# Start and end of an attention plus two gated-layer kernel: new order of the first three chunks, last outputs stored bank by bank

## The chip, the cores and the metric

The kernel runs on one core of a Trainium2 chip. The time is the device time of one execution in microseconds (us); lower is better. A time is given as the median of several runs.

## The reference

```python
def _attn_ref(q, k, v, alpha):          # B, H, S, D = 4, 8, 768, 48
    for t in range(S):
        state = alpha[:, :, t, :, None] * state + np.einsum('bhd,bhe->bhde', k[:, :, t], v[:, :, t])
        y[:, :, t] = np.einsum('bhd,bhde->bhe', q[:, :, t], state)
# x = y as 3072 tokens x 384
x = (1 / (1 + np.exp(-(x @ w_gate)))) * (x @ w_val) @ w_out           # d_ff 1536
h = np.maximum(np.maximum(x @ w1, x @ w2), x @ w3)                     # d_ff 768
out = (h @ w_out2).astype(np.float32)
```

alpha lies between 0.8 and 1.0, so the kernel's general path (for an alpha further than 0.25 from 1) is compiled in but not executed for these inputs.

## The kernel before, in words

**Tiling.** The 3072 tokens are 24 chunks of 128 (CH) for the attention, 8 tiles of 384 (three chunks) for layer 1 and 6 tiles of 512 for layer 2. A chunk's attention is done in parallel form: running products of alpha (`scans`, `recips` on VectorE) scale q and k (`scale_qk`), TensorE computes `scores`, VectorE masks them (`masked`), TensorE transposes k (`transposes`), ScalarE copies the transposed keys to SBUF (`khs_copy`), TensorE forms the chunk's update of the state (`outer`) and the output y of the chunk (`attend`: the masked scores times v and, but for the first chunk of a batch, q times the state), VectorE updates the state (`new_state`), and ScalarE copies y to `x_raw` (`y_copy`). Part of y has the wrong rows; it is copied to `y_last` and moved by six small SBUF to SBUF transfers per tile (`move_last`, 24 KB each, two for each third k of the features, counted by `last_moved[k]`). Then every operand is split into a high and a low fp32r part (`x_split` on ScalarE gives `x_hi`, `x_rest` on VectorE gives `x_lo`), and every product is three passes of TensorE (`product`, L927, and `out1`, `out2`).

**Order.** Each engine has its own hand-written program; semaphores tie them. The attention of the chunks of tile T+1 lies between the products of tile T. Only the attention of the first three chunks (tile 0) has nothing beside it: it is the start of the kernel, L792 to L813 on VectorE, L1010 to L1022 on TensorE, L551 to L571 on ScalarE, L321 to L333 on SP (the queue that issues the loads). Layer 1 of tile 0 starts when `x_hi` of k = 0 is there.

**Places that the change touches.**

- `ps_y` (L108), the PSUM region of y, is one region for all chunks, across the two banks of `ps_pair`. So `attend` (L905) waits for `y_evac`: y of chunk 1 must be copied out before `attend(2, 0)` may write. `y_slot` (L901) picks a head's place in it.
- TensorE's order at the start (L1010 to L1022) is scores 0, transposes 0, outer 0, attend 0, scores 1, transposes 1, outer 1, scores 2, transposes 2, attend 1, outer 2, attend 2.
- ScalarE's order (L551 to L571) is key copy 0, `split_w1(0)`, y 0, `split_w1(1)`, key copy 1, `check(0)`, key copy 2, y 1, `check(1)`, y 2, two of the small moves (L565, from ScalarE's own queue, k = 1), `split_w1(2)`, and the three `x_split`. `check` (L538) tests alpha in two activations and gives `viol_done`.
- SP's order (L326 to L333) is w1 1 to 4, chunk 4, chunk 3, w1 5, the four moves of k = 0 and 2, w1 6 and on. `load_chunk(4)` waits for `y_done` 1 and `viol_done` 1, `load_chunk(3)` for `y_done` 2 and `viol_done` 2 (L236), `load_w1(5)` for `y_done` 2, and a chunk is two transfers, alpha (256 KB, L241) and the rest (704 KB, L242).
- VectorE's order (L806 to L811) is masked 1, new_state 1, masked 2, new_state 2, x_rest. Then `layer1` (L696) begins with `scans` and `recips` of chunk 3, ahead of the multiplication that gives the first h (L717).
- GpSimd makes the low parts of the weights (`split_first`, `split_w1`) and scales q and k of chunks 3 to 5 in between (L391 to L399).
- At the end, `out2` (L1029) does 12 matmuls: for each of the three passes n, all four banks s. `o_done` comes with the last one, then ScalarE copies the four banks (`o_copy`, L595) and SP stores each copy, 192 KB (L353 to L355).
- The general path, `general` and `slow_layers` on each engine, stands behind a branch on a flag.

Of the kernel before, what the change touches and what calls it, by code (L numbers as in the profile page):

```python
# [24 lines left out]
F32 = mybir.dt.float32  # L25
F32R = mybir.dt.float32r
I32 = mybir.dt.int32
ALU = mybir.AluOpType
# [35 lines left out]
def build(nc, att_in, vT, w1, w2, consts, y, out):  # L64
    with ExitStack() as ctx:
# [6 lines left out]
        def sem(name):  # L72
# [29 lines left out]
        ps_gate = pb("ps_gate", [P, 512])  # L102
        ps_val = pb("ps_val", [P, 512])
# [4 lines left out]
        ps_y = ps_pair[:, 512 - 2 * CH:512 + 2 * CH].rearrange("p (s t) -> p s t", s=PAIRS)  # L108
# [29 lines left out]
        o_evac, stored = sem("o_evac"), sem("stored")  # L138
        gen_qka, gen_v, gen_kv, gen_st, gen_prod = (sem(n) for n in ("gen_qka", "gen_v", "gen_kv", "gen_st", "gen_prod"))
        gen_sum, gen_row, gen_stored, gen_fix = sem("gen_sum"), sem("gen_row"), sem("gen_stored"), sem("gen_fix")  # L140
        s_w_in, s_w_hi, s_w_lo = sem("s_w_in"), sem("s_w_hi"), sem("s_w_lo")
        s_x_hi, s_x_lo, s_gate, s_val, s_sig, s_h = (
            sem(n) for n in ("s_x_hi", "s_x_lo", "s_gate", "s_val", "s_sig", "s_h"))
        s_h_hi, s_h_lo, s_out, s_mid = sem("s_h_hi"), sem("s_h_lo"), sem("s_out"), sem("s_mid")
        s2_w_in, s2_w_hi, s2_w_lo = sem("s2_w_in"), sem("s2_w_hi"), sem("s2_w_lo")
        s2_x_hi, s2_x_lo, s2_abc, s2_a, s2_ab, s2_h = (
            sem(n) for n in ("s2_x_hi", "s2_x_lo", "s2_abc", "s2_a", "s2_ab", "s2_h"))
        s2_h_hi, s2_h_lo, s2_out, s2_evac, s2_stored = (
            sem(n) for n in ("s2_h_hi", "s2_h_lo", "s2_out", "s2_evac", "s2_stored"))
# [42 lines left out]
        def arrived(eng, sems, Cs, i):  # L192

            if Cs == 2:
                eng.wait_ge(sems[2], 16)
            elif Cs < 2:
                eng.wait_ge(sems[Cs], 16)
            else:
                eng.wait_ge(sems[Cs % 2], (Cs // 2 + Cs % 2 + 3 * i) * 16)

# [31 lines left out]
        def _(sp):  # L232
# [58 lines left out]
            def slow_layers():  # L291
                for f in range(NF1):
                    if f > 0:
                        sp.wait_ge(s_w_hi, f)
                        sp.wait_ge(s_w_lo, f)
                    sp.dma_start(inbuf[:, 0:W1C], w1[f]).then_inc(s_w_in, 16)
                with sp.Fori(0, B) as b:
                    for half in (0, 1):
                        T = b * 2 + half
                        sp.wait_ge(s_x_lo, T * KT + 1)  # L300
                        for k in range(KT):
                            for r in (0, 1):
                                (p, n0), (pl, nl) = head_at(r, k), head_at(r, KT)
                                for n, (row, src) in enumerate((
                                        (ODD * r, y[b * PAIRS + p, n0, :, half * TOK:(half + 1) * TOK]),
                                        (ODD * r + D, y[b * PAIRS + pl, nl, GAP * k:GAP * (k + 1),
                                                        half * TOK:(half + 1) * TOK]))):
                                    sp.dma_start(x_raw[row:row + (GAP if n else D), k, :], src).then_inc(gen_fix, 16)
                sp.wait_ge(s_out, TILES * NF1 + 1)
                for j in range(NF2):  # L310
                    if j > 0:
                        sp.wait_ge(s2_w_hi, j)
                        sp.wait_ge(s2_w_lo, j)
                    sp.dma_start(inbuf[:, INC:INC + W2C], w2[j]).then_inc(s2_w_in, 16)
                sp.sem_inc(s2_stored, 16)
                with sp.Fori(0, TILES2) as T:
                    sp.wait_ge(s2_evac, T * SUB + 2 * SUB)
                    sp.dma_start(out[T], stage_out).then_inc(s2_stored, 16)
                sp.wait_ge(s2_stored, TILES2 * 16 + 16)
# [94 lines left out]
        def _(act):  # L414
# [13 lines left out]
            def y_copy(Cs, i):  # L428
# [6 lines left out]
                t = slice(c * CH, (c + 1) * CH)  # L435
# [59 lines left out]
            def slow_layers():  # L495
                act.sem_inc(s_sig, 1)
                act.sem_inc(s_mid, KT)
                for f in range(NF1):
                    act.wait_ge(s_w_in, 16 * (f + 1))
                    copy(w_hi[:, f * W1C:(f + 1) * W1C], inbuf[:, 0:W1C]).then_inc(s_w_hi, 1)  # L500
                with act.Fori(0, TILES) as T:
                    act.wait_ge(gen_fix, T * (4 * KT * 16) + 4 * KT * 16)
                    act.wait_ge(s_out, T * NF1 + 1)
                    for k in range(KT):
                        copy(x_hi[:, k, 0:TOK], x_raw[:, k, :]).then_inc(s_x_hi, 1)
                    for f in range(NF1):
                        act.wait_ge(s_gate, T * NF1 + f + 1)
                        act.wait_ge(s_h, T * NF1 + f + 1)
                        nc.scalar.activation(act_sb[:, :], ps_gate[:, 0:TOK], ACT.Sigmoid).then_inc(s_sig, 1)
                        act.wait_ge(s_h, T * NF1 + f + 2)  # L510
                        act.wait_ge(s_out, T * NF1 + f + 1)
                        copy(h_hi[:, 0, 0:TOK], h_sb[:, :]).then_inc(s_h_hi, 1)
# [3 lines left out]
                for j in range(NF2):  # L516
                    act.wait_ge(s2_w_in, 16 * (j + 1))
                    copy(w_hi[:, j * W2C:(j + 1) * W2C], inbuf[:, INC:INC + W2C]).then_inc(s2_w_hi, 1)
                act.sem_inc(s2_a, 1)
                act.sem_inc(s2_evac, SUB)  # L520
                with act.Fori(0, TILES2) as T:
                    act.wait_ge(s2_out, T * NF2 + 1)
                    act.wait_ge(s_mid, TILES * KT + KT)
                    for k in range(KT):
                        copy(x_hi[:, k, :], mid_tile2(T, k)).then_inc(s2_x_hi, 1)
                    for f in range(NF2):
# [3 lines left out]
                        act.wait_ge(s2_h, T * NF2 + f + 2)  # L530
                        act.wait_ge(s2_out, T * NF2 + f + 1)
                        copy(h_hi[:, 0, :], h2).then_inc(s2_h_hi, 1)
# [27 lines left out]
            check(1, 0)  # L560
# [32 lines left out]
            layer1(TILES - 1, 0, False, True, {LAST_READ[j] + 2: split_w2(j) for j in range(NF2)})  # L593

# [32 lines left out]
            o_copy(TILES2 - 1)  # L627
# [7 lines left out]
        def _(dve):  # L635
# [105 lines left out]
            def slow_layers():  # L741
                dve.sem_inc(s_h, 1)
                dve.sem_inc(s_x_lo, 1)
                dve.sem_inc(s2_h, 1)
                for f in range(NF1):
                    dve.wait_ge(s_w_hi, f + 1)
                    a = slice(f * W1C, (f + 1) * W1C)
                    nc.vector.tensor_tensor(w_lo[:, a], inbuf[:, 0:W1C], w_hi[:, a].bitcast(F32),
                                            ALU.subtract).then_inc(s_w_lo, 1)
                with dve.Fori(0, TILES) as T:  # L750
                    for k in range(KT):
                        dve.wait_ge(s_x_hi, T * KT + k + 1)
                        nc.vector.tensor_tensor(x_lo[:, k, 0:TOK], x_raw[:, k, :], x_hi[:, k, 0:TOK].bitcast(F32),
                                                ALU.subtract).then_inc(s_x_lo, 1)
                    for f in range(NF1):
                        dve.wait_ge(s_val, T * NF1 + f + 1)
                        dve.wait_ge(s_sig, T * NF1 + f + 2)
                        nc.vector.tensor_tensor(h_sb[:, :], act_sb[:, :], ps_val[:, 0:TOK], ALU.mult).then_inc(s_h, 1)
                        dve.wait_ge(s_h_hi, T * NF1 + f + 1)
                        nc.vector.tensor_tensor(h_lo[:, 0, 0:TOK], h_sb[:, :], h_hi[:, 0, 0:TOK].bitcast(F32),  # L760
                                                ALU.subtract).then_inc(s_h_lo, 1)
                for j in range(NF2):
                    dve.wait_ge(s2_w_hi, j + 1)
                    a = slice(j * W2C, (j + 1) * W2C)
                    nc.vector.tensor_tensor(w_lo[:, a], inbuf[:, INC:INC + W2C], w_hi[:, a].bitcast(F32),
                                            ALU.subtract).then_inc(s2_w_lo, 1)
                with dve.Fori(0, TILES2) as T:
                    for k in range(KT):
                        dve.wait_ge(s2_x_hi, T * KT + k + 1)
                        nc.vector.tensor_tensor(x_lo[:, k, :], mid_tile2(T, k), x_hi[:, k, :].bitcast(F32),  # L770
                                                ALU.subtract).then_inc(s2_x_lo, 1)
                    for f in range(NF2):
                        dve.wait_ge(s2_a, T * NF2 + f + 2)
# [410 lines left out]
```

## Time and profile before

| what | value |
|---|---|
| median of 3 runs | 874.21 us (873.68 to 874.39) |
| the profiled execution, its own time | 872.64 us |
| span of its profile | 870.8 us |
| TensorE (PE) busy | 847.7 us, 97% |
| VectorE, ScalarE, GpSimd busy | 353.5, 279.3, 114.1 us |
| instructions recorded | 14019 |

The span runs from the first to the last instruction of the profiled execution; 1.84 us of its own time lie around it. PE, DVE, ACT and POOL are TensorE, VectorE, ScalarE and GpSimd; PEld is TensorE's weight load, which runs beside its matmuls. SPq and ACTq are the issuing of transfers on the two queues. A name such as L922 is a line of the code above; L416 is the copy helper of ScalarE, used by many steps.

### The profile page before, as it was taken

Reading aid. Unit: us, or ns where it says so; the run is one execution under the profiler, and the core shown is the slowest. Engines: PE = TensorE matmul, PEld = TensorE weight load, DVE = VectorE, ACT = ScalarE, POOL = GpSimd, SP = SyncE. Lnnn points to the kernel's source line nnn. Section 1 sums busy time; section 2 is a strip of 40 time slices with the busy share of each in tenths; the row PEclk is TensorE's granted clock in tenths of the full one; section 3 lists DMA queues with packets and bytes.
Section 4 is the critical chain, followed back from the end, with each engine's and each line's share of the span. In section 5 each row is a group of like instructions: output and inputs, shape, how many; then the busy total and the mean of one; then the engine's idle time right before and its main releaser. Section 6 shows DMA issues by size and latency. Waiting matters only on the chain.

```text
span 870.8 us, 14019 instructions
## 1 busy us (share of the span) xinstructions
PE 847.7 (97%) x5565; PEld 786.1 (90%) x5565; DVE 353.5 (41%) x660; ACT 279.3 (32%) x520; POOL 114.1 (13%) x88
## 2 busy tenths in 40 slices
PE   5699999999999999999999999999999999999997
PEld 4599999999999999999999999988888888888886
DVE  7364354364274265255255322232323232232321
ACT  3364433333343333333333334421312122131211
POOL 1266121021012011012011004400000000000000
PEclk9999999999999999999999999999999999999999
DMA  7350210200111111021021022100100100000001
GB/s 279 124 209 1 99 46 1 99 18 30 54 44 47 40 59 47 8 91 47 5 93 47 1 80 78 69 1 1 37 1 0 36 0 36 0 36 0 36 0 39
DMA packets 14452, 42.17 MB, mean 48 GB/s; under 512 B 1984, under 2 KB 5952, under 8 KB 14400
## 3 DMA queue, kind: packets, MB, share of 16 engines
q1 hardware_dynamic: 14336, 41.38, 13.4%
q8 instruction: 39, 0.64, 0.3%
q14 instruction: 13, 0.11, 0.0%
q10 hardware_dynamic: 64, 0.05, 0.0%
HBM read 35.52 MB, written 4.72 MB: 46 GB/s over the span
## 4 chain that ended last, share of the span: by engine, by line
PE 97%; DVE 1%; DMA 1%; issue 0%; ACT 0%; SPq 0%; DVEq 0%; ACTq 0%
PE ps_out L959 18%; PE ps_gate L934 17%; PE ps_val L934 17%; PE ps_gate L940 9%; PE ps_val L940 9%; PE ps_out L1041 6%; PE ps_sc L934 6%; PE ps_pair L922 3%; PE ps_sc L940 3%; PE ps_sc L886 3%; PE ps_pair L1041 2%; PE ps_pair L918 1%; PE ps_pair L870 1%; PE ps_sc L896 1%; DMA x_raw<-x_raw 1%
## 5 line engine op out<-in xcount | busy, mean ns | idle before, releaser
L934 PE MATMUL ps_gate<-x_hi,w_hi 128*128 128x384 f32 (+1 forms) x396 | 139.7, 353 | 7.0 <-ACT x_hi L416 7.0
L934 PE MATMUL ps_val<-x_hi,w_hi 128*128 128x384 f32 (+1 forms) x396 | 140.6, 355 | 0.0
L934 PE MATMUL ps_gate<-x_hi,w_lo 128*128 128x384 f32 (+1 forms) x396 | 139.1, 351 | 0.0
L934 PE MATMUL ps_val<-x_hi,w_lo 128*128 128x384 f32 (+1 forms) x396 | 138.7, 350 | 0.0
L717 DVE TENSOR_TENSOR h_sb<-act_sb,ps_val 128x384 f32<-128x384 f32 x96 | 53.0, 552 | 169.1 <-PE ps_val L940 168.1
L940 PE MATMUL ps_gate<-x_lo,w_hi 128*128 128x384 f32 (+1 forms) x396 | 118.1, 352 | 0.0
L940 PE MATMUL ps_val<-x_lo,w_hi 128*128 128x384 f32 (+1 forms) x396 | 117.1, 349 | 0.0
L416 ACT ACTIVATE h_hi<-h_sb 128x384 fp32r<-128x384 f32 x96 | 50.4, 525 | 150.2 <-DVE h_sb L717 150.1
L462 ACT ACTIVATE act_sb<-ps_gate 128x384 f32<-128x384 f32 x96 | 47.2, 491 | 132.5 <-PE ps_gate L940 132.5
L934 PEld LDWEIGHTS ps_gate<-x_hi,w_hi 128*128 128x128 f32 x396 | 74.7, 189 | 10.6 <-issue 7.4
L836 DVE TENSOR_TENSOR probs<-probs,ps_val 128x512 f32<-128x512 f32 x36 | 24.7, 687 | 137.8 <-PE ps_val L940 137.8
L693 DVE TENSOR_TENSOR h_lo<-h_sb,h_hi 128x384 fp32r<-128x384 f32 x96 | 58.1, 605 | 52.0 <-ACT h_hi L416 52.0
L934 PEld LDWEIGHTS ps_val<-x_hi,w_hi 128*128 128x128 f32 x396 | 74.7, 189 | 4.4
L934 PEld LDWEIGHTS ps_val<-x_hi,w_lo 128*128 128x128 f32 x396 | 74.7, 189 | 4.4
L940 PEld LDWEIGHTS ps_gate<-x_lo,w_hi 128*128 128x128 f32 x396 | 73.4, 189 | 5.1
L934 PEld LDWEIGHTS ps_gate<-x_hi,w_lo 128*128 128x128 f32 x396 | 74.8, 189 | 3.2
L940 PEld LDWEIGHTS ps_val<-x_lo,w_hi 128*128 128x128 f32 x396 | 73.1, 188 | 4.2
L959 PE MATMUL ps_out<-h_hi,w_hi 128*128 128x384 f32 x288 | 67.9, 343 | 0.0
L959 PE MATMUL ps_out<-h_hi,w_lo 128*128 128x384 f32 x288 | 65.6, 335 | 0.0
L959 PE MATMUL ps_out<-h_lo,w_hi 128*128 128x384 f32 x288 | 65.4, 334 | 0.0
L369 POOL TENSOR_TENSOR inbuf<-inbuf,decay 112x512 f32<-112x512 f32 x21 | 27.1, 1292 | 288.5 <-DVE decay L645 284.8
L416 ACT ACTIVATE h_hi<-probs 128x512 fp32r<-128x512 f32 x36 | 22.8, 633 | 130.5 <-DVE probs L840 130.4
(113 smaller groups left out, 1242.2 us busy)
## 6 DMA issues: line engine op xcount, KB each, us to landing
inbuf<-att_in SPq DMA_DIRECT2D x23, 704.0 KB, 5.1
mid<-w SPq DMA_DIRECT2D x12, 576.0 KB, 7.3
inbuf<-att_in SPq DMA_DIRECT2D x23, 256.0 KB, 2.7
inbuf<-w SPq DMA_DIRECT2D x6, 768.0 KB, 4.3
out<-inbuf SPq DMA_DIRECT2D x5, 768.0 KB, 3.5
x_raw<-x_raw SPq DMA_DIRECT2D x46, 24.0 KB, 1.9
out<-inbuf SPq DMA_DIRECT2D x4, 192.0 KB, 2.4
mid<-att_in SPq DMA_DIRECT2D x1, 704.0 KB, 8.5
```

The lines of the kernel that those rows point to most:

```text
L369: nc.gpsimd.tensor_tensor(att(buf(Cs), Q), att(buf(Cs), Q), decay[0:PR, par], ALU.mult).then_inc(qh_done, 1)
L416: return nc.scalar.activation(o, i_, ACT.Copy)
L462: nc.scalar.activation(act_sb[:, :], ps_gate[:, 0:TOK], ACT.Sigmoid).then_inc(sig_done, 1)
L693: nc.vector.tensor_tensor(h_lo[:, f % 2, 0:w], h, h_hi[:, f % 2, 0:w].bitcast(F32), ALU.subtract).then_inc(lo_done, 1)
L717: nc.vector.tensor_tensor(h_sb[:, :], act_sb[:, :], ps_val[:, 0:TOK], ALU.mult).then_inc(h_done, 1)
L836: nc.vector.tensor_tensor(act2, act2, ps_val[:, :], ALU.max).then_inc(ab_done, 1)
L886: ins = mm(bank[:, p * CH:(p + 1) * CH], att(buf(Cs), K, r)[:, p, :], att(buf(Cs), Q, r)[:, p, :], start=True, stop=True)
L922: ins = mm(y_slot(p, n), v_cols(buf(Cs), (2 * p + n) * D, D), probs_of(Cs, i)[:, PAIRS * n + p, :], start=(first and p < 2), stop=True, sk ...
L934: mm(bank, w_at(half, f, c + k * P, total=total), x_hi[:, k, 0:w], start=(k == 0 and half == 0), stop=False)
L940: return mm(bank, w_at(0, f, c + k * P, total=total), x_lo[:, k, 0:w], start=False, stop=(k == KT - 1))
L959: ins = mm(ps_out[:, m, 0:TOK], w_at(wh, f, 2 * DM + m * P), h[:, f % 2, 0:TOK], start=(f == 0 and n == 0), stop=(f == NF1 - 1 and n == 2))
L1041: ins = mm(out_bank[s][:, 0:DM], h[:, f % 2, s * P:(s + 1) * P], w_at(wh, f, 3 * DM, DM, W2C), start=(f == 0 and n == 0), stop=(f == NF2 - ...
```

## The change

The edits:

1. y of chunk 1 gets its own banks (`ps_gate`, `ps_val`, now one tensor `ps_gv`), so `attend` of the first tile waits for no y copy but `attend(2)` for the one of chunk 0; the wait of `attend` for `khs_done` stays only outside the first tile, as before.
2. TensorE's `attend(0, 0)` goes behind scores and transposes of chunk 1. ScalarE's key copy 1 goes ahead of y 0. VectorE's `new_state(1)` goes behind the masks of chunk 2.
3. SP issues the four small moves ahead of chunk 3 and w1 5; ScalarE does `check(1)` behind its two moves (it was ahead of y 2), and `split_w1(2)` behind the three `x_split`.
4. The last `out2` runs bank by bank: three matmuls of a bank, then the next bank, each bank with its own count of `o_last`; ScalarE copies each bank on its count.
5. The general path's `slow_layers` are rewritten with loops and plain fp32 products (not executed here, and left out of the diff below); the kernel has 12 semaphores fewer for it and one more, `o_last`.

```diff
-        ps_gate = pb("ps_gate", [P, 512])
-        ps_val = pb("ps_val", [P, 512])
+        ps_gv = pb("ps_gv", [P, 2 * 512])
+        ps_gate, ps_val = ps_gv[:, 0:512], ps_gv[:, 512:1024]
...
-        ps_y = ps_pair[:, 512 - 2 * CH:512 + 2 * CH].rearrange("p (s t) -> p s t", s=PAIRS)
...
+        def y_banks(Cs, i):
+
+            two = ps_gv if isinstance(i, int) and Cs == 1 else ps_pair
+            return two[:, 512 - 2 * CH:512 + 2 * CH].rearrange("p (s t) -> p s t", s=PAIRS)
...
@@ SP @@
             load_chunk(4, 0)
+            move_last(0, (0, 2))
             load_chunk(3, 0)
-            load_w1(RING - 3)
-            move_last(0, (0, 2))
-            for f in range(RING - 2, NF1):
+            for f in range(RING - 3, NF1):
                 load_w1(f)
...
@@ ScalarE @@
             act.wait_ge(consts_in, 16)
+            khs_copy(1, 0)
             y_copy(0, 0)
             split_w1(1)
-            khs_copy(1, 0)
             check(0, 0)
             khs_copy(2, 0)
             y_copy(1, 0)
-            check(1, 0)
             y_copy(2, 0)
             act.wait_ge(y_evac, CPT - 1)
             act.wait_ge(last_evac, 1)
             for r in (0, ODD):
                 act.dma_start(x_raw[r + D:r + D + GAP, 1, :],
                               y_last[r + GAP:r + 2 * GAP, :]).then_inc(last_moved[1], 16)
-            split_w1(2)
+            check(1, 0)
             act.wait_ge(y_evac, CPT)
             for k in range(KT):
                 act.wait_ge(last_moved[k], 32)
                 x_split(0, k, x_raw[:, k, :])
+            split_w1(2)
...
+            def o_copy_last():
+                act.wait_ge(stored, 16 * (TILES2 - 1))
+                for s in range(SUB):
+                    act.wait_ge(o_last, s + 1)
+                    copy(stage_out[:, s, :], out_bank[s][:, 0:DM]).then_inc(o_evac, 1)
...
-            o_copy(TILES2 - 1)
+            o_copy_last()
...
@@ VectorE @@
             masked(1, 0, 0)
             masked(1, 0, 1)
-            new_state(1, 0)
             masked(2, 0, 0)
             masked(2, 0, 1)
+            new_state(1, 0)
             new_state(2, 0)
...
@@ TensorE @@
-                if not (isinstance(i, int) and Cs == 0):
+                if not (isinstance(i, int) and Cs < CPT):
                     pe.wait_ge(y_evac, C)
-                if not (isinstance(i, int) and Cs < CPT):
                     pe.wait_ge(khs_done, C + 1)
+                elif Cs == 2:
+                    pe.wait_ge(y_evac, 1)
...
             outer(0, 0)
-            attend(0, 0)
             scores(1, 0)
             transposes(1, 0)
+            attend(0, 0)
             outer(1, 0)
...
-            out2(TILES2 - 1, NF2 - 1)
+            pe.wait_ge(h2_hi_done, TILES2 * NF2)
+            pe.wait_ge(h2_lo_done, TILES2 * NF2)
+            f = NF2 - 1
+            for s in range(SUB):
+                for n, (h, wh) in enumerate(((h_hi, 0), (h_hi, 1), (h_lo, 0))):
+                    ins = mm(out_bank[s][:, 0:DM], h[:, f % 2, s * P:(s + 1) * P],
+                             w_at(wh, f, 3 * DM, DM, W2C), start=False, stop=(n == 2))
+                ins.then_inc(o_last, 1)
```

## Rows read from the trace of the kernel before

**Rows 1.** The page, part 2: busy tenths of TensorE in 40 slices of 21.8 us.
```profile
PE   5699999999999999999999999999999999999997
```

**Rows 2.** Chain of waits, 0 to 60 us, in order: start us, us, what.
```profile
13.56 1.95 PE ps_pair L922 x16
...
19.09 0.88 PE ps_sc L896 x10
19.97 2.01 PE ps_out L886 x16
21.98 0.94 PE ps_out L870 x4
22.92 1.03 PE ps_pair L918 x16
...
25.83 0.64 PE ps_out L896 x16
...
27.18 1.11 PE ps_pair L918 x16
...
30.22 0.27 ACT x_raw L416
...
30.84 0.64 SPq L263
...
36.46 0.53 ACT x_hi L416
37.12 1.62 PE ps_gate L934 x4
...
40.34 1.28 PE ps_val L934 x4
...
42.53 0.69 PE ps_gate L934 x4
...
57.25 1.01 PE ps_pair L922 x16
```

**Rows 3.** Timeline, 0 to 40 us: start us, us, engine, line, operation.
```profile
11.79 0.88 PE L896 MATMUL ps_out<-inbuf,khs 128*48 128x48 f32 x16 [0.63 <-ACT khs L416]
...
17.63 0.68 DVE L790 TENSOR_TENSOR mid<-mid,rdec 112x512 f32<-112x512 f32 x1
...
25.89 1.20 ACT L416 ACTIVATE x_raw<-ps_pair 48x512 f32<-48x512 f32 x2 [2.38 <-PE ps_pair L922]
27.11 0.72 ACT L542 ACTIVATE inbuf<-inbuf,cst 128x512 f32<-128x512 f32 x1
...
28.49 0.19 ACT L545 ACTIVATION_READ_ACCUMULATOR inbuf<-inbuf,cst 128x1 f32 x1
...
32.42 1.16 ACT L416 ACTIVATE w_hi<-mid 128x1152 fp32r<-128x1152 f32 x1 [0.64 <-issue]
```

**Rows 4.** Tile x_raw, 26 to 37 us: landing of its six moves.
```profile
DMA to landing us min/median/max: 3.8/4.6/5.0
```

**Rows 5.** Tile x_raw, 80 to 240 us: landing of 18 later moves.
```profile
DMA to landing us min/median/max: 1.8/1.9/3.5
```

**Rows 6.** Transfers issued 26 to 37 us: KB each, median us to landing.
```profile
inbuf<-att_in SPq DMA_DIRECT2D x1, 256.0 KB, 2.6
x_raw<-x_raw ACTq DMA_DIRECT2D x2, 24.0 KB, 4.8
```

**Rows 7.** Timeline of VectorE, 26 to 100 us.
```profile
38.42 1.36 DVE L645 TENSOR_TENSOR_SCAN decay<-inbuf,zero 112x128 f32<-112x128 f32 x4
...
42.57 0.55 DVE L717 TENSOR_TENSOR h_sb<-act_sb,ps_val 128x384 f32<-128x384 f32 x1 [1.09 <-PE ps_val L940]
```

**Rows 8.** Chain of waits, 862 to 871 us.
```profile
865.84 0.49 ACT inbuf L416
```

**Rows 9.** Stores to out and waits of SP, 860 to 871 us.
```profile
L355 SPq DMA_DIRECT2D out<-inbuf x4: 354/438/458, 866.4 to 867.7; - x4
...
SPq L65 <- DMA out<-inbuf: 2.2, 1, 2.2
```

More of the change, by code:

```diff
@@ L291, in slow_layers @@
             def slow_layers():
[L292 to L314, printed above, removed]
+                with sp.Fori(0, TILES) as T:
+                    b, t0 = T // 2, T % 2 * TOK
+                    sp.wait_ge(s_out, T * NF1 + 1)
+                    for k in range(KT):
+                        for r in (0, 1):
+                            (p, n), (pl, nl) = head_at(r, k), head_at(r, KT)
+                            sp.dma_start(x_raw[ODD * r:ODD * r + D, k, :],
+                                         y[b * PAIRS + p, n, :, bass.ds(t0, TOK)]).then_inc(gen_fix, 16)
+                            sp.dma_start(x_raw[ODD * r + D:ODD * r + D + GAP, k, :],
+                                         y[b * PAIRS + pl, nl, GAP * k:GAP * (k + 1), bass.ds(t0, TOK)]).then_inc(gen_fix, 16)
+                    with sp.Fori(0, NF1) as f:
+                        sp.wait_ge(s_out, T * NF1 + f + 1)
+                        sp.dma_start(w_slow, w1[f]).then_inc(s_w_in, 16)
@@ L315, in slow_layers @@
                 sp.sem_inc(s2_stored, 16)
                 with sp.Fori(0, TILES2) as T:
+                    with sp.Fori(0, NF2) as f:
+                        sp.wait_ge(s2_out, T * NF2 + f + 1)
+                        sp.dma_start(w2_slow, w2[f]).then_inc(s2_w_in, 16)
                     sp.wait_ge(s2_evac, T * SUB + 2 * SUB)
@@ L521, in slow_layers @@
                 with act.Fori(0, TILES2) as T:
[L522 to L526, printed above, removed]
+                    with act.Fori(0, NF2) as f:
                         act.wait_ge(s2_abc, T * NF2 + f + 1)
@@ L762, in slow_layers @@
[L762 to L766, printed above, removed]
-                with dve.Fori(0, TILES2) as T:
[L768 to L773, printed above, removed]
+                with dve.Fori(0, TILES) as T:
+                    with dve.Fori(0, NF1) as f:
+                        g = T * NF1 + f
+                        dve.wait_ge(s_val, g + 1)
+                        dve.wait_ge(s_sig, g + 2)
+                        dve.wait_ge(s_out, g + 1)
+                        nc.vector.tensor_tensor(h_sb[:, :], act_sb[:, :], ps_val[:, 0:TOK], ALU.mult).then_inc(s_h, 1)
@@ new lines, in slow_layers, with whole, step1, step2 @@
+            def slow_layers():
+                def whole(bank, w, c, x):
+                    for k in range(KT):
+                        ins = mm(bank, w[:, c + k * P:c + (k + 1) * P], x(k), start=(k == 0), stop=(k == KT - 1))
+                    return ins
+                def step1(T, f):
+                    g, first = T * NF1 + f, isinstance(f, int)
+                    pe.wait_ge(s_w_in, g * 16 + 16)
+                    pe.wait_ge(s_sig, g + 1)
+                    whole(ps_gate[:, 0:TOK], w_slow, 0, lambda k: x_raw[:, k, :]).then_inc(s_gate, 1)
+                    pe.wait_ge(s_h, g + 1)
+                    whole(ps_val[:, 0:TOK], w_slow, DM, lambda k: x_raw[:, k, :]).then_inc(s_val, 1)
+                    pe.wait_ge(s_h, g + 2)
+                    for m in range(KT):
+                        ins = mm(ps_out[:, m, 0:TOK], w_slow[:, 2 * DM + m * P:2 * DM + (m + 1) * P], h_sb[:, :],
+                                 start=first, stop=True, skip_group_check=True)
+                    ins.then_inc(s_out, 1)
+                def step2(T, f):
+                    G, first = T * NF2 + f, isinstance(f, int)
+                    pe.wait_ge(s2_w_in, G * 16 + 16)
+                    pe.wait_ge(s2_h, G + 1)
+                    whole(ps_gate[:, :], w2_slow, 0, lambda k: mid_tile2(T, k))
+                    whole(ps_val[:, :], w2_slow, DM, lambda k: mid_tile2(T, k))
+                    whole(ps_sc[:, :], w2_slow, 2 * DM, lambda k: mid_tile2(T, k)).then_inc(s2_abc, 1)
+                    pe.wait_ge(s2_h, G + 2)
+                    for s in range(SUB):
+                        ins = mm(out_bank[s][:, 0:DM], h2[:, s * P:(s + 1) * P], w2_slow[:, 3 * DM:4 * DM],
+                                 start=first, stop=True, skip_group_check=True)
+                    ins.then_inc(s2_out, 1)
@@ L1118, in _ @@
+                    step2(T, 0)
+                    with pe.Fori(1, NF2) as f:
+                        step2(T, f)
             pe.wait_ge(flag_ready, 1)
```

111 lines of the change are left out of this document (24 added, 87 removed).

## The prediction

> **What bounds the kernel now.** I read the page's slices first [rows 1]: TensorE is busy in nine tenths or more from the third slice to the last but one. Between about 44 and 863 us it is the bound, and no edit touches what it does there. Only the start (until layer 1 begins) and the last few us can change, so I read the chain of waits for both, in order of time.
>
> At the start the chain is on TensorE from the masks of chunk 0 to the end of `attend(2)` [rows 2]. Then come y copy, the issue of a small move, its landing (until 36.4), `x_split` at 36.46 and the first product at 37.12. So the start has two parts: TensorE's attention work with its holes, and the road of the last y rows by way of a transfer. At the end the chain is last matmul, four copies [rows 8], four stores, landing [rows 9].
>
> **Durations against medians.** The sum is made against the profiled execution, 872.64 us (span 870.8 and 1.84 around it). That is 1.57 below the median of the three runs; I subtract the same gain from 874.21.
>
> **Part 1, TensorE's order (edits 1 and 2).** `outer(0)` ends at 11.79 + 0.88 = 12.67 [rows 3]. Before, TensorE then waits for the masks until 13.56, later as long for key copy 1 as it did for key copy 0 (0.63 [rows 3]), and from 26.47 to 27.18 for the y copy of chunk 1, which `attend(2)` needed [rows 2]. In the new order its work after 12.70 is: scores 2.01, transposes 0.94, attend 1.95, outer 0.88, scores 2.01, transposes 0.94, attend with state 25.83 - 22.92 = 2.91, outer 0.64, attend 30.22 - 27.18 = 3.04 [rows 2]. (Scores and transposes of chunk 1 have the shapes of chunk 2.) Sum 15.32, end 28.02 where it was 30.22: **2.2 us earlier**, if no wait is left. I go through them:
> - scores 1 needs k of chunk 1, scaled before 12.67 (VectorE masks chunk 0 behind it and is done before 13.56).
> - Key copy 1 now runs beside `attend(0)` (from 15.7, done 16.3); outer 1 starts at 17.6.
> - scores 2 would start at 18.48; k of chunk 2 is scaled at 17.63 + 0.68 = 18.31 [rows 3]. Cover 0.17 us, the thinnest one; each us that VectorE is later costs a us.
> - Key copy 2: ScalarE has y 0 (1.20), w1 1 (1.16) and check 0 (1.57) between 17.6 and 21.6 [rows 3]; transposes 2 end at 21.4, the copy is done at 22.2, outer 2 needs it at 24.35.
> - `new_state(1)` moves behind the masks of chunk 2 (21.9, or 22.7 if GpSimd slows VectorE there) and ends by 23.5; attend(2) needs it at 24.98. Edit at nothing, cover 1.5 us.
> - chunk 4's load starts 1 us later, since `check(0)` ends at 21.6; its 960 KB are through by about 27, ahead of the moves.
>
> **Part 2, the moves (edit 3).** From the end of `attend(2)` to the first SP move it takes 30.84 - 30.22 = 0.62, so the moves issue from 28.64. ScalarE spends 32.42 - 30.84 = 1.58 until its two issues are over [rows 2, 3], so until 30.22, and then has `check(1)`: 28.49 + 0.19 - 27.11 = 1.57 [rows 3], until 31.8. For the landing: before, the six moves took 3.8 to 5.0 [rows 4], while chunk 3 and w1 5 (1.5 MB) were issued directly ahead. Later moves with nothing ahead land in 1.9, 1.8 to 3.5 [rows 5]. I take 1.9, since after the edit nothing is queued ahead either. k = 0 is there at 28.64 + 0.64 + 1.9 = 31.2; k = 2 at 30.6 + 1.9 = 32.5. So `x_split` 0 starts when `check(1)` ends, at 31.8 instead of 36.46: **4.66 us earlier in all** (2.2 of it part 1). The check in that place costs 0.6 against the landing at 31.2. With landings of 3.5, it starts at 32.8 (gain 3.7).
>
> Here a rule speaks against this reading. The trace shows ScalarE's own moves, on the other queue, landing in 4.8, as late as SP's [rows 6]. The Trainium skill, "DMA: Bandwidth & Descriptors", section "Queues, rings and completion order", says that a transfer engine takes turns between queues packet by packet; by that alone ScalarE's two moves should not have stood behind SP's bulk, so something else (their small rows) would have made them slow, and they would stay slow. By the rule the gain of this part is nil (first rival); by the later moves it is the one above.
>
> What is passed by the moves: SP issues chunk 3 only after `check(1)`, at 31.85, and w1 5 behind it. Alpha of chunk 3 lands after 2.6 [rows 6], at 34.5. VectorE ends `x_rest` at 38.42 - 4.66 = 33.8 and waits 0.7. It was idle 1.09 before the first h [rows 7], so h is not late. If it were: h was done at 43.12 [rows 7], and the value product of f = 1, which is the first to wait for it, comes nine matmuls of 0.17 after 42.53, at 44.1 [rows 2], so another 1.0 is free. Alpha may land until 33.8 + 1.09 + 1.0 = 35.9. Cost 0, bound 1 us. w1 5 is first read at f = 5, several steps later. `split_w1(2)` behind the x_splits ends by 34.5 and GpSimd's low part some 3 us later; f = 2 comes a whole step after f = 1, which starts at 42.53 - 4.66 = 37.9. Nothing.
>
> **Clock.** Layer 1 starts at half pace: four matmuls take 1.28 at 40.34 and 0.69 at 42.53 [rows 2], so the 4.5 us to 41.6 cost some 2.1 more than at full pace. The attention before it is at half pace too (1.95 against 1.01 at 57.25 [rows 2]). The profile's granted clock reads full all along, so it is the pitch that tells. I keep the 2.1; this stretch may be shorter or longer, from 0 to 4.2, and I allow 1 us either way.
>
> **Part 3, the end (edit 4).** Before, the copies start at 865.84 after the last matmul, SP's last issue is at 867.7 and the landing is waited for 2.2 more [rows 8, 9]. Now three copies are done when the last bank is, and its copy ends at 865.84 + 0.5 = 866.35; the last issue is then at 866.38, 1.35 earlier. The stores before were squeezed together; now they come 0.5 apart, which the data of each just fits, so the landing may be up to 0.5 shorter. **1.6 us** (1.3 to 1.9).
>
> **Edit 5** is not executed: 0. Nearest bound is the 1.84 us around the span; nothing of a smaller program shows in a row, so 0.3 either way.
>
> **Sum.** 4.66 + 1.6 = 6.3. 872.64 - 6.3 = 866.3 for such an execution, and **867.9** as a median.
>
> **Rivals.**
> - *The moves are slow by themselves.* They take 5.62 from issue to `x_split` as before: 28.64 + 5.62 = 34.26, gain 2.2 + 1.6 = 3.8, time 870.4. For it: ScalarE's queue was as slow [rows 6]. Against: 1.9 for 18 later ones [rows 5]. 0.08.
> - *TensorE's clock rises in the denser start.* Its work is now unbroken for 15.3 us; before, it was unbroken for 7.4 (19.09 to 26.47) and still at half pace. If it rises at the same 7.4 (20.1), the other 7.9 us of part 1 shrink by 1.01/1.95 to 4.1: 3.8 more, 864.1. Against: both long stretches before stayed slow. The Trainium skill, "TensorE: Matmul & The Clock Gate", "What's actually happening", says that sustained busy time raises the clock, which speaks for this; the trace so far does not follow it. 0.06.
> - *The change doesn't do what it says*: a wait left in the first tile (k of chunk 2, or key copies) holds TensorE as before, and the moves wait for chunk 4. Then only the end is gained and perhaps some tenths: 872.6 or so. 0.05.
> - *Slower: chunk 3 comes too late.* VectorE stands in `scans` of chunk 3 with the first h queued behind it, and TensorE stands for h. From alpha at 35.9 on each us costs one. Slower by over 0.2% needs it 6.3 + 1.75 later, at 43.95, 12 us after its issue, where 2.6 was seen. 0.02.
> - *In between*: alpha or landings somewhat late, 869 to 870.5. 0.07.
> - The forecast: 0.72.
>
> **How the numbers follow.** A measurement of this kernel can tell about 0.2% (1.75 us) from no change. Faster: 0.72 + 0.08 + 0.06 + 0.07 = 0.93; same 0.05; slower 0.02. Range: bounds of 1 us of the clock, 0.9 of the landings, 0.3 of the end; upward it also takes in the first rival at 870.4. 866.0 to 870.5 leaves out the clock's rise, the third and fourth rival and some of the tails.
>
> **What would show it.** Right: `attend(2)` ends near 28.0, moves of the first tile land in about 2, `x_split` starts at 31.8 at the end of `check(1)` and the first product at 32.5; VectorE waits a little for alpha before L645; the last store is issued 0.6 after the last matmul. Wrong: landings of 4 or more; a hole in TensorE before scores 2; TensorE idle after its first product; L922 at 1.0 instead of 1.9 before 30 us.

## The result and the profile after

| | before | after |
|---|---|---|
| median | 873.94 us (870.71 to 874.39, 4 runs) | 864.59 us (864.26 to 864.84, 4 runs) |
| profiled execution: own time, span | 872.64, 870.8 us | 864.78, 863.0 us |

The ratio is 0.990, 95% interval 0.9882 to 0.9919: 9.3 us faster by the medians, 7.9 by the two profiled executions. The forecast was 867.9 in a range from 866.0 to 870.5, so the direction was right and the gain 3 us larger than I had it, and the time lies below the range. (The kernel before has a fourth run here, 870.71, which moves its median from 874.21 to 873.94.)

The page of the changed kernel, part 1 (busy us, share of the span, instructions):

```profile
PE 842.9 (98%) x5565; PEld 782.3 (91%) x5565; DVE 354.7 (41%) x660; ACT 279.1 (32%) x520; POOL 114.1 (13%) x88
```

The work is the same, and TensorE is busy 4.8 us less for the same 5565 matmuls. That can't come from waits removed; some of its matmuls ran faster. The chain of waits of the changed kernel, 0 to 60 us (start us, us, what):

```profile
15.64 1.91 PE ps_pair L882 x15
17.57 0.59 ACT x_raw L409
...
22.04 0.56 PE ps_out L855 x16
22.60 0.59 PE ps_pair L878 x16
23.19 1.04 PE ps_pair L882 x15
24.25 0.27 ACT x_raw L409
...
27.84 0.20 ACT inbuf L519
28.09 2.60 DMA inbuf<-att_in
...
33.35 1.04 DVE decay L625 x3
...
35.97 0.53 DVE h_sb L697
36.55 0.97 PE ps_gv L894 x4
```

L882 is the product with v in `attend`: 1.91 for chunk 0, 1.04 for chunk 2, at 23.19 already. The same product took 1.95 before and 1.01 only at 57 us [rows 2]. TensorE's own timeline shows where the pace changes:

```profile
17.30 0.80 PE L855 MATMUL ps_sc<-inbuf,khs 128*48 128x48 f32 x16
18.49 1.16 PE L845 MATMUL ps_out<-mid 48*128 48x128 f32 x16 [0.39 <-DVE mid L749]
19.59 0.60 PE L829 MATMUL ps_out<-cst,mid 112*128 112x112 f32 x4
```

Scores of chunk 2 (L845) take 1.16, where they took 2.01 [rows 2]. So the clock went from its lower level (1.2 GHz) to the upper (2.4) near 18 us, after TensorE had worked from 11.81 with no stand longer than 0.4 us. `attend(2)` ended at 24.24 and not at 28.0. The moves landed as forecast, 1.8 to 2.2 after their issue where it was 3.8 to 5.0 [rows 4] (tile x_raw, 20 to 36 us, changed kernel):

```profile
DMA to landing us min/median/max: 1.8/1.9/2.2
```

`x_split` started at 27.93, with the end of `check(1)`, and the first product at 28.58, 8.5 us earlier. Not all of it lasted. VectorE's and GpSimd's timelines, 26 to 38 us:

```profile
30.71 3.66 DVE L625 TENSOR_TENSOR_SCAN decay<-inbuf,zero 112x128 f32<-112x128 f32 x4 [0.75 <-DMA inbuf<-att_in]
...
35.97 0.52 DVE L697 TENSOR_TENSOR h_sb<-act_sb,ps_gv 128x384 f32<-128x384 f32 x1
```

```profile
30.48 2.66 POOL L372 TENSOR_TENSOR w_lo<-mid,w_hi 128x1152 fp32r<-128x1152 f32 x1 [4.39 <-ACT w_hi L409]
```

The four scans of chunk 3, which took 1.36 [rows 7], take 3.66 beside GpSimd's `split_w1(2)`. They are not slower all through. The first alone takes 2.71, from 30.71 to 33.42, just past the end of GpSimd's operation (33.14), and the other three 0.39 each (VectorE's timeline, 30.6 to 31.2 us):

```profile
30.71 2.71 DVE L625 TENSOR_TENSOR_SCAN decay<-inbuf,zero 112x128 f32<-112x128 f32 x1 [0.75 <-DMA inbuf<-att_in]
```

So it looks as if the scan stood until GpSimd was done. h is late and TensorE stands 1.65 us for it. From the output product of f = 0 to the last matmul everything is shifted by one amount: the last matmul ends at 858.54, and the copies behind it began at 865.84 before, 7.3 us.

The end: stores to out, SP's last wait, and the chain, 850 to 863 us of the changed kernel:

```profile
L348 SPq DMA_DIRECT2D out<-inbuf x4: 355/401/1349, 857.6 to 859.9; - x4
```

```profile
SPq L65 <- DMA out<-inbuf: 2.1, 1, 2.1
```

```profile
858.56 0.49 ACT inbuf L409
```

The last copy ends at 859.05, as planned, but SP's third issue, from 858.55, took 1.35 instead of 0.44 [rows 9], so the last store was issued at 859.9, 1.4 after the last matmul and not 0.6. From the last matmul to the end of the span it is 4.5 us; it was 5.0.

### The profile page after: what moved, and what is told of

Same layout as the page of the kernel before. It is cut to its first block, busy times and chain, and to the rows that moved or that the text cites. A ratio compares the mean times of both kernels' runs of the same rounds, so it can differ in the third digit from the quotient of the medians.

```text
span 863.0 us, 14018 instructions
## 1 busy us (share of the span) xinstructions
PE 842.9 (98%) x5565; PEld 782.3 (91%) x5565; DVE 354.7 (41%) x660; ACT 279.1 (32%) x520; POOL 114.1 (13%) x88
## 4 chain that ended last, share of the span: by engine, by line
PE 96%; ACT 1%; DVE 1%; issue 1%; DMA 1%; ACTq 0%; DVEq 0%; SPq 0%
PE ps_gv L894 34%; PE ps_out L919 18%; PE ps_gv L900 17%; PE ps_out L1001 6%; PE ps_sc L894 6%; PE ps_sc L900 3%; PE ps_pair L882 3%; PE ps_sc L845 3%; PE ps_pair L1001 2%; PE ps_pair L829 1%; PE ps_pair L878 1%; PE ps_sc L855 1%; DMA inbuf<-att_in 1%; DVE decay L625 0%; ACT x_raw L409 0%
## 5 line engine op out<-in xcount | busy, mean ns | idle before, releaser
L894 PE MATMUL ps_gv<-x_hi,w_hi 128*128 128x384 f32 (+1 forms) x792 | 280.3, 354 | 6.0 <-ACT x_hi L409 4.4
L894 PE MATMUL ps_gv<-x_hi,w_lo 128*128 128x384 f32 (+1 forms) x792 | 277.7, 351 | 0.0
L900 PE MATMUL ps_gv<-x_lo,w_hi 128*128 128x384 f32 (+1 forms) x792 | 235.3, 351 | 0.0
L894 PEld LDWEIGHTS ps_gv<-x_hi,w_hi 128*128 128x128 f32 x792 | 149.3, 189 | 14.2 <-issue 4.6
L894 PEld LDWEIGHTS ps_gv<-x_hi,w_lo 128*128 128x128 f32 x792 | 149.3, 189 | 7.5
L900 PEld LDWEIGHTS ps_gv<-x_lo,w_hi 128*128 128x128 f32 x792 | 146.5, 188 | 9.3
L697 DVE TENSOR_TENSOR h_sb<-act_sb,ps_gv 128x384 f32<-128x384 f32 x96 | 52.9, 551 | 167.8 <-PE ps_gv L900 167.1
L637 DVE TENSOR_TENSOR_SCAN rdec<-inbuf,rdec,zero 112x127 f32<-112x127 f32 x92 | 60.7, 691 | 0.8
L919 PEld LDWEIGHTS ps_out<-h_hi,w_lo 128*128 128x128 f32 x288 | 51.6, 188 | 0.0
L919 PEld LDWEIGHTS ps_out<-h_lo,w_hi 128*128 128x128 f32 x288 | 51.3, 188 | 0.0
```

Source lines behind the costliest of these rows:

```text
L637: nc.vector.tensor_tensor_scan(rdec[0:PR, par, p, CH - 2::-1], att(buf(Cs), ALPHA)[:, p, CH - 1:0:-1], zero[0:PR, :].broadcast_to([PR, CH ...
L894: mm(bank, w_at(half, f, c + k * P, total=total), x_hi[:, k, 0:w], start=(k == 0 and half == 0), stop=False)
L900: return mm(bank, w_at(0, f, c + k * P, total=total), x_lo[:, k, 0:w], start=False, stop=(k == KT - 1))
L919: ins = mm(ps_out[:, m, 0:TOK], w_at(wh, f, 2 * DM + m * P), h[:, f % 2, 0:TOK], start=(f == 0 and n == 0), stop=(f == NF1 - 1 and n == 2))
```

## The experiments

Theory A: TensorE's clock rose because the new order has no stand just before it; the 3 us beyond the forecast are this. Theory B: chance. Later a third, that the mix of operations of the new order does it.

**Part by part.** `e_order` has edits 1 and 2 on the kernel before, `e_moves` edit 3 alone, `e_tail` edit 4 alone; their diffs are those parts of the diff above. `e_attend0_first` is the changed kernel with

```diff
             outer(0, 0)
+            attend(0, 0)
             scores(1, 0)
             transposes(1, 0)
-            attend(0, 0)
             outer(1, 0)
```

> The kernel before with the banks of chunk 1 and the new order of TensorE, ScalarE's key copy and VectorE's state alone; SP's order, check(1), the moves and the end are those of before. Theory A (TensorE's unbroken work at the start lifts its clock): scores of chunk 2 take about 1.2 us instead of 2.0, attend(2) ends near 24.3, the moves stand behind chunk 3 and w1 5 and land in 4 to 5 us, x_split near 31: 5.4 us faster, about 868.6. Theory B (that the clock rose in the changed kernel is chance of the run): attend(2) ends near 28, 2.2 us faster, 871.8, in most runs.

> The kernel before with edit 3 alone (small moves ahead of chunk 3 and w1 5, check(1) behind ScalarE's moves, split_w1(2) behind the x_split). If the moves were late because of the bulk ahead of them they land in about 2 us; x_split starts when check(1) ends, 30.84 + 1.58 + 1.57 = 34.0 instead of 36.5: 2.4 us faster, 871.6. If their small rows make them slow, they still land in 4 to 5 us and nothing is gained. TensorE's clock in the start as before (scores 2 in 2.0 us) by theory A; by theory B it may rise in some runs.

> The kernel before with the last products bank by bank alone. By the sum 1.6 us faster, 872.4. In the changed kernel the last store was issued 1.4 us after the last matmul instead of 0.6, with one issue of 1.35 us. If that long issue comes with this edit (SP, ScalarE and TensorE closer together at the end), this run shows it too and gains 0.6 us; if it belongs to the changed program as a whole, this run gains 1.3 to 1.6.

> The changed kernel with attend of chunk 0 ahead of scores and transposes of chunk 1 again, all else as changed. TensorE waits again for the masks of chunk 0 (0.9 us) and for key copy 1 (0.6 us). Theory A: with these holes the clock does not rise before layer 1, attend(2) ends near 28.5, 4 us slower than the changed kernel, about 868.6. Theory B: only the two holes cost, 1.5 us at most, about 866.

Measured, beside 31 runs of the kernel before (median 873.73):

| run | median us | ratio, 95% | landing of the six moves |
|---|---|---|---|
| e_order | 871.13 | 0.999 (0.997 to 1.001) | 4.6 to 6.2 |
| e_moves | 870.91 | 0.9975 (0.9952 to 0.9997) | 1.8 to 2.2 |
| e_tail | 873.26 | 0.9997 (0.9973 to 1.0021) | 4.6 to 7.0 |
| e_attend0_first | 868.20 | 0.9943 (0.9924 to 0.9963) | 1.9 to 2.2 |

The kernel before turned out to have two groups of times: of the 31 runs 11 lie between 869.2 and 870.8 and 20 between 873.2 and 875.0. That makes ratios to it coarse; what stands in the profiles is clearer. The changed kernel was not run again beside the later ones. `e_old_general` below, which differs from it only in code that is not executed, gave 864.61 against 864.59 on such a later occasion; no other run checks that the occasions compare.

`e_order`: scores of chunk 2 took 1.16 and `attend(2)` ended at 24.06, 6.2 us earlier than before, so the order alone lifts the clock. But ScalarE, still with `check(1)` ahead of y 2, began the y copy only at 24.63, and the moves stood behind the bulk (tile x_raw, 20 to 40 us of `e_order`). `x_split` began at 32.72 (forecast 31), so 3.7 of the 6.2 were left, and the time is a miss: 871.13 where 868.6 was expected.

```profile
DMA to landing us min/median/max: 4.6/5.3/6.2
```

`e_moves` has the old order and the landings of the changed kernel. With `e_order` it settles the first rival: the moves are slow only behind the bulk. It does not settle its own time, since it has VectorE's late h too (value product of f = 1 at 41.16, behind a stand of 1.39 us).

`e_tail` gained 0.5 by the medians where 1.6 was expected, with no ratio clear of 1; its profile has a long issue too, of 0.88 us. The three parts alone give 2.6, 2.8 and 0.5 us, 5.9 in all, and together 9.1 against the same median: the new order pays in full only when the moves need not wait for the bulk.

`e_attend0_first` gives the old order in a kernel with all other edits: scores of chunk 2 take 2.01 again (chain of waits, 11 to 45 us), and it is 3.6 us slower than the changed kernel. Theory A had said 4.0, theory B 1.5 at most. Not every run agrees: of its ten, eight lie between 867.4 and 869.3, but two are 865.4 and 865.9, as theory B had it; the profiled one ran 869.0.

```profile
19.03 0.88 PE ps_sc L855 x16
19.91 2.01 PE ps_out L845 x16
...
25.77 0.64 PE ps_out L855 x16
26.41 1.03 PE ps_pair L878 x16
```

**Which stand.** `e_before_filled` keeps the old order and fills its holes with repeated scores; `e_one_hole` and `e_late_hole` have the new order and one stand each:

```diff
# e_before_filled, on the kernel before
             outer(0, 0)
+            again(0, (0, 1), (ps_gate, ps_val))
             attend(0, 0)
             scores(1, 0)
             transposes(1, 0)
+            again(1, (0,), (ps_out[:, 0, :], ps_out[:, 2, :]))
             outer(1, 0)
# e_one_hole, on the changed kernel
             outer(0, 0)
+            pe.wait_ge(mask_done, 2)
             scores(1, 0)
# e_late_hole, on the changed kernel
             attend(0, 0)
+            pe.wait_ge(kh_done, 2 * CPT)
             outer(1, 0)
```

> The kernel before, its order unchanged, with the two holes of TensorE's start filled: scores of pairs 0 and 1 of chunk 0 computed again behind outer 0, and of pair 0 of chunk 1 behind transposes 1 (the results are not used). Theory A (unbroken work lifts the clock, whatever its order): scores of chunk 2 take 1.2 us instead of 2.0 and attend 1 and 2 run at full pace, the first product starts 3 us or less earlier (the y copy of chunk 1 and the bulk ahead of the moves remain), 871 to 872 and no longer two groups of times. Theory C (it needs the new order, its mix of operations): half pace as before until 27 us or later.

> The changed kernel with one wait added: TensorE waits for the masks of chunk 0 before scores of chunk 1, so that the hole of 0.9 us of the old order is back and the order is the new one. Hole theory: the clock stays at half through scores 2 (2.0 us) and the time is 3 to 4 us longer, as with attend 0 first (868). Order theory (the mix of operations before 18 us lifts the clock): scores 2 take 1.2 us, the time grows by the 0.9 us of the hole, less what the rest hides, 865.0 to 865.5.

> The changed kernel with one wait: outer of chunk 1 waits for k of chunk 2, so that TensorE stands 0.8 us from 17.6, about where the old order stood 0.6 us for key copy 1. Late-hole theory: with it the clock does not rise at 18 to 19 us, scores 2 take 2.0 us at 19.2 and the time is that of the old order in the changed kernel, 868. Order theory: scores 2 take 1.2 us in spite of the hole, the time grows by 0.8 us at most, 865.4.

`e_before_filled`: 871.75 us (0.9989, 0.9969 to 1.001), still in two groups. Its timeline of TensorE is neither expectation: scores of chunk 1 fell from 0.21 to 0.11 a pair at 15.6, so the clock did rise once the first hole was filled. Then TensorE, through with its transposes earlier than before, had to wait for key copy 1, which ScalarE began at 17.96 behind y 0 and w1 1. TensorE stood 1.07 us, and the granted clock fell to half (windows: us, PE, PEld, DVE, ACT and POOL busy, PEclk, DMA share, GB/s):

```profile
18.55 0.86 PE L896 MATMUL ps_sc<-inbuf,khs 128*48 128x48 f32 x16 [1.07 <-ACT khs L416]
```

```profile
18.00:20.00 2.00, 1.45 (x22) 1.36 (x24) 1.85 (x5) 1.93 (x4) 1.72 (x2) 0.66 0.00 0
20.00:22.00 2.00, 2.00 (x18) 1.77 (x16) 0.99 (x2) 0.00 (x0) 1.32 (x2) 0.50 0.43 126
```

`e_one_hole`: 865.60 us, 1.0 more than the changed kernel, which is the stand itself; scores of chunk 2 took 1.57, so the clock rose within them (TensorE's timeline).

```profile
19.09 1.57 PE L845 MATMUL ps_out<-mid 48*128 48x128 f32 x16
```

`e_late_hole`: 867.50 us, 2.9 more; three of its four runs were within 867.47 to 867.63 and one was 865.03. Same order, a stand of 0.88 us ahead of outer 1, and half pace until about 25:

```profile
18.34 0.88 PE L855 MATMUL ps_sc<-inbuf,khs 128*48 128x48 f32 x16 [0.88 <-DVE mid L749]
19.15 2.08 PE L845 MATMUL ps_out<-mid 48*128 48x128 f32 x16
```

So it is the stand of TensorE at 17.5 us and not the mix of operations. A stand of about the same length at 12.7 did little; the work after it was unbroken.

But place and length of a stand do not settle it alone. `e_best` (below) stood 1.08 us at the same place, and its scores of chunk 2 still took 1.16, with a granted clock of 1.00 throughout (its timeline of TensorE):

```profile
15.46 1.49 PE L884 MATMUL ps_pair<-probs,inbuf 128*48 128x128 f32 x16
...
18.39 1.16 PE L847 MATMUL ps_out<-mid 48*128 48x128 f32 x16 [1.08 <-DVE mid L751]
```

There the clock had risen before the stand, within the product of `attend(0)` (1.49, where all 16 at half pace take 1.95). In the changed kernel it rose just behind that product, and in `e_no_general`, whose TensorE does the same work up to there, only in scores 2 (1.21). So the moment of the rise differs from run to run, by some 2 us here, and a stand at 17.5 holds the clock down if it comes first. `e_late_hole`'s fourth run and the two short ones of `e_attend0_first` would fit this; none of them was profiled. Why a stand of 1.07 brought a raised clock down in `e_before_filled`, and one of 1.08 in `e_best` did not, stays open.

**What was lost in layer 1.** `e_split2_early` moves one step of ScalarE, `e_awake` adds work for TensorE:

```diff
# e_split2_early
             y_copy(1, 0)
+            split_w1(2)
             y_copy(2, 0)
...
                 x_split(0, k, x_raw[:, k, :])
-            split_w1(2)
# e_awake
             attend(2, 0)
+            pe.wait_ge(w_hi_done, 1)
+            for n in range(23):
+                mm(ps_out[:, 0, 0:TOK], w_hi[:, 0:P], w_hi[:, 0:TOK], start=True, stop=True)
             layer1(0, 0, True, False, {})
```

> The changed kernel with ScalarE's split_w1(2) between the y copies of chunk 1 and chunk 2 instead of behind the x_splits. In the changed kernel the four scans of chunk 3 took 3.66 us instead of 1.36, with GpSimd's low part of w1 2 (30.48 to 33.14) beside them, the first h came at 35.97 and TensorE stood 1.65 us. If GpSimd's work beside them is the cause, it now runs before alpha of chunk 3 arrives, the scans take 1.4, TensorE does not stand and the time is 1.5 us shorter, about 863.1. If late alpha is the cause (rival), the scans stay long and nothing is gained.

> The changed kernel with 23 matmuls of 384 columns added (their result is not used) where TensorE waits for the moves of the first tile. Theory: TensorE's granted clock falls to half while it stands, so that layer 1 starts at half pace for 3 us. With the added work the first product's matmuls follow each other in 0.17 us instead of 0.32 and the value product of f = 0 ends 1.5 us earlier, but the first h waits for VectorE's scans anyway, so the time changes by less than 0.3 us, 864.6. If the clock in the first us of a product is always low, 0.32 stays.

`e_split2_early`: 863.29 us, 1.3 less. The scans are back at 1.38 (VectorE's timeline) with the same wait for alpha before them (0.77), so alpha was not the cause, and TensorE does not stand for h. Its profiled run, 864.1, is its slowest of four; layer 1 was at half pace until 33.5 in it, 2 us longer than in the changed kernel.

```profile
30.47 1.38 DVE L625 TENSOR_TENSOR_SCAN decay<-inbuf,zero 112x128 f32<-112x128 f32 x4 [0.77 <-DMA inbuf<-att_in]
```

`e_awake`: 865.83 us, 1.2 more, a miss. Layer 1 did start at full pace, but its h was as late as before (35.97), TensorE stood for it 2.97 us instead of 1.65, and the clock fell behind that stand, in the output product of f = 0 (chain, and windows as above):

```profile
38.55 2.88 PE ps_out L919 x9
```

```profile
38.00:40.00 2.00, 2.00 (x9) 2.00 (x8) 1.66 (x4) 0.79 (x3) 1.53 (x3) 0.52 0.00 0
```

**The end.** `e_no_general` leaves out the general path, with the reading of its flag and the branches on every engine. `e_last_on_act` lets ScalarE issue the last store. `e_old_tail` is the changed kernel with the old end, `e_old_general` the one with the old general path.

```diff
# e_last_on_act: SP's loop over the last stores ends one earlier, and in o_copy_last
+                act.wait_ge(o_evac, TILES2 * SUB)
+                act.dma_start(out[TILES2 - 1][:, SUB - 1, :], stage_out[:, SUB - 1, :]).then_inc(stored, 16)
```

> The changed kernel without the general path, the reading of its flag and its branches on all engines. If SP's long issue near the end (1.35 us) comes from the loading of code behind the branches that TensorE and ScalarE take at that moment, it is gone, the last store is issued 0.6 after the last matmul and the time is 0.8 us shorter, 863.8. If it comes from stores in flight, it stays.

> The changed kernel with the last of the four stores issued by ScalarE behind its own copy. SP's long issue then holds up nothing but the third store; the last is issued 0.6 us after the last matmul's end plus the issue on ScalarE's queue, some 0.8 us earlier than now: about 863.9. If the long issue is a stall of the transfer engines for all queues, ScalarE's issue is long too and nothing is gained.

> The changed kernel with the end of the kernel before (the twelve last matmuls pass by pass, copies behind the last). If the end gained 1.6 us as forecast, 866.2. By the two profiles (last matmul to end of span 5.0 before, 4.5 now) it gained 0.5, so 865.1; by kernels with the old end whose last landing was waited for 2.9 to 3.6 us instead of 2.2, up to 1.5, 866.1.

> The changed kernel with the general path of the kernel before, all other edits made. If the compact path gives nothing, 864.6. If the smaller program takes part in the gain beyond the forecast (fewer or shorter code loads at the end), it is slower by up to 1 us, 865.6, and the long issue of SP or the wait for the last landing is longer in its profile.

`e_no_general`: 863.26 us, 1.3 less. Its four issues took 0.33 to 0.36 each, the last landing was waited for 1.6, and no instruction packets moved in that stretch:

```profile
SPq L65 <- DMA out<-inbuf: 1.6, 1, 1.6
```

So the long issue goes with the general path and its branches. That the loading of code behind them is what holds it up is argued, not shown. In the changed kernel an instruction packet moved at 858.2 to 858.4, just ahead of the long issue, and none during it; before, one moved at 867.8, amid the four issues, and none of them was longer than 0.46. `e_old_tail` has the branches and the old end, and its longest issue took 0.62. `e_last_on_act`: 864.12, 0.5 less (expected 0.7). `e_old_tail`: 865.23, so edit 4 gave 0.6 of the 1.6 forecast. `e_old_general`: 864.61, so edit 5 gave nothing.

**The kernel before again.** Four more profiles of it, to see its two groups:

> The kernel before once more, for its start. Its times lie in two groups, near 870 and near 874. Theory: in the group near 870 the clock rises at about 27 us, within attend(2), and in the other it does not rise before layer 1, so that attend(2) and more of layer 1 run at half pace. This look shows which one it is and its time.

> The kernel before, a further look, to meet a run of its group near 870. If it is one, its clock has risen before 20 us or layer 1 starts at full pace, 3 to 4 us less of half pace than in the two profiles near 873 and 874; if the group has another cause, the start looks like theirs.

> The kernel before, a further look, to meet a run of its group near 870. If it is one: either its clock rises before 20 us (attend 1 and 2 in 1.0 us) or the last landing is short; if near 874, half pace until 25 us or later and a wait of 3 us or more for the last landing.

> The kernel before, one more look, with the same two outcomes: near 870 with the clock up before 20 us or with a short last landing, or near 874 with half pace until 25 us or later and a wait of 3 us or more at the end.

They ran 874.1, 873.8, 873.62 and 874.68; none was of the group near 870, so what sets that group apart stays open. (In all, 18 of 71 runs of this kernel lie near 870.) In three of the four the clock rose at about 25 to 27 us and `attend(2)` ended 1.4 to 1.7 us earlier than in the profile I predicted from, yet `x_split` began at 36.2 to 36.8 all the same, since the moves still stood behind the bulk. That refutes my first thought about the groups: a rise at 27 is no gain in this kernel. The wait for the last landing was 3.5, 3.2, 3.8 and 3.2 us; the profile I had shows 2.2 [rows 9] (the longest, `e_before_look3`):

```profile
SPq L65 <- DMA out<-inbuf: 3.8, 1, 3.8
```

**All together.** `e_best` is the changed kernel with `e_split2_early`, `e_awake` and `e_last_on_act`.

> The changed kernel with the three edits that were tried alone: split_w1(2) early (1.3 us), the 23 added matmuls (layer 1 at full pace, 1.5 us now that VectorE is not late) and the last store issued by ScalarE (0.5 us): 864.6 - 3.3 = 861.3. If the clock falls later because TensorE stood, as with the added matmuls alone, it should not here, since nothing stands; if it falls all the same, 862.5 or more.

861.27 us (861.13 to 861.45, 5 runs), ratio 0.9865 (0.9842 to 0.9888): 3.3 us below the changed kernel, as summed. The first product starts at 28.48 and takes 0.94 for four matmuls, then 0.17 each, and nothing stands afterwards. The added matmuls, which lost 1.2 us alone, are worth 1.5 once h is in time, if the other two steps keep their worth of 1.3 and 0.5; no run has those two without them.

## Why the prediction was wrong

- **Part 1, removed waits: right.** TensorE's order, the covers of key copies and of `new_state`, and scores 2 right behind k of chunk 2 (18.49 against 18.48 in the sum) came as worked out. That 18.49 meets the sum so well is partly luck: by then TensorE was faster than in the sum and stood 0.39 us for k of chunk 2, and later 0.26 for key copy 2.
- **Clock: the step that failed.** The prediction took every duration of part 1 at half pace ("The attention before it is at half pace too") and gave a rise in the denser start 0.06, with 3.8 us and 864.1. That rival is what happened: `attend(2)` ended at 24.24 instead of 28.02, and the time is 864.6. Its 3.8 us came out with some luck, since the rise came near 18 and not at 20.1, and stands of 0.39 and 0.26 us took part of it back; the time is near its 864.1 because the terms below pull both ways. My argument against it was that 7.4 us of unbroken work before had stayed at half pace. It took the moment of the rise from one profile. In three of the four further profiles of the same kernel the clock rose at 25 to 27 us, so the half pace that I had read up to 30 was no property of that kind of work. By the Trainium skill, "TensorE: Matmul & The Clock Gate", "What's actually happening", sustained busy time raises the clock; the runs here agree with it (1.16 for scores 2 in the changed kernel, 2.01 with a stand of 0.9 us ahead), and I should have given it more.
- **Part 2, the moves: right.** Landing 1.9 was taken and 1.8 to 2.2 measured, `x_split` at the end of `check(1)`, 3.7 us after the y copy began (3.8 in the sum). By the Trainium skill, "DMA: Bandwidth & Descriptors", "Queues, rings and completion order", a transfer engine takes turns between queues, so ScalarE's moves should not have waited for SP's bulk. The measurement decides against that reading here: 4.8 before [rows 6], at most 2.2 with no bulk ahead.
- **Part 2, "h is not late, cost 0, bound 1 us": wrong, 1.3 us.** I had let `split_w1(2)` pass as hidden and counted only when its result is read, not that a scan of VectorE may stand until GpSimd's operation beside it is done (3.66 for the four scans, against 1.38 with it moved away).
- **Layer 1's half pace**, 4.5 us before [rows 2], was 3.0 in the changed kernel (28.58 to 31.6), worth some 0.7 (half of the 1.5 us between them); within the 1 us allowed.
- **Part 3, the end: mis-sized.** 1.6 forecast, 0.6 by `e_old_tail`. The copies came as worked out; one issue of 1.35 us did not. `e_tail`, on the kernel before, gained 0.5 by the medians.
- **Profile against median.** I moved the gain over to the median unchanged. The profile's wait of 2.2 for the last landing was no usual one; in four others it is 3.2 to 3.8. That would be about 1 us of the 1.4 between the gain of the medians and that of the profiles; no run separates it, and the rest is not accounted for.

## What to carry to other kernels

An engine whose pace depends on its own recent work has no fixed price per instruction: where an edit closes its stands, price the same work at both levels and give both a real chance, even if the trace before shows only one. And a step moved into idle time is not free when another engine is slowed beside it: a scan on VectorE that takes 0.39 us took 2.71 beside a GpSimd operation, as it stood until that was done. A remedy may cost alone and pay with another: the added matmuls lost 1.2 us while h was late and gained when it was not.

## What the runs showed that I had not expected

- What a stand of TensorE costs depends on where it lies: 0.9 us of standing at 12.7 us cost 1.0 us of time, the same at 17.5 us cost 2.9, since the clock then stayed at its lower level until about 25 us. With the clock already up, 1.08 us at the same place did not bring it down in `e_best`, though 1.07 did in `e_before_filled`.
- The profile's granted clock reads 1.00 in the start of all these kernels, also where the matmuls go at half pace; it shows half only after a fall (0.50 at 20 to 22 us of `e_before_filled`). The pitch of the matmuls is the surer sign.
- An issue of a store took 1.35 us instead of 0.4 near the end, and 0.88 to 1.76 in the other kernels with the new end and the general path; without that path and its branches none was longer than 0.36.
- One kernel can have two groups of times 4 us apart with identical work (before: 870 and 874) and its neighbour none (the changed kernel: 864.3 to 864.8 in four runs; `e_order`: 869.7 to 871.6 in ten). Runs 2 to 4 us below the others turned up only in kernels in which TensorE stands ahead of `outer(1)`, as in `e_moves` (3 of 10) and `e_attend0_first` (2 of 10). That points at the clock, but no such run was profiled.
